# A fused attention and two-layer feed-forward kernel: GpSimd alone makes the fold's forms, and the big output stage's small operations are reordered

## The reference

```
x = attention(q, mean of k over 8, mean of v over 8)      # 2304 tokens x 512
x = x / rms(x) * rms_g
h = silu(x @ w_gate) * (x @ w_val)                        # 512 -> 1536, FFN 1
x = h @ w_out                                             # 1536 -> 512
out = silu(x @ w2_in) @ w2_out                            # 512 -> 2048 -> 512, FFN 2
```

## Time and profile before

| | us |
|---|---|
| median of 3 runs | 895.41 (895.05 to 895.97) |
| profiled execution, its own time | 899.02 |
| its span, first to last instruction | 897.2 |
| TensorE busy | 872.5 |
| VectorE busy | 520.8 |
| ScalarE busy | 356.9 |
| GpSimd busy | 336.5 |

### The profile page before, as it was taken

The page is one execution under the profiler, slowest core; times in us unless marked ns, Lnnn a source line. Parts: engine busy times, 40 slices in busy tenths (PEclk is TensorE's granted clock), DMA queues, the critical chain, the costliest instruction groups (busy, mean ns, idle before and its releaser), DMA issues.

```text
span 897.2 us, 12951 instructions
## 1 busy us (share of the span) xinstructions
PE 872.5 (97%) x4896; PEld 828.2 (92%) x4896; DVE 520.8 (58%) x831; ACT 356.9 (40%) x671; POOL 336.5 (38%) x345
## 2 busy tenths in 40 slices
PE   7999999999989999999999999998999999999998
PEld 6899999999889999999898999898989998989897
DVE  6689757765456766655654355668555544433433
ACT  3679744542243432355453212134234332322222
POOL 6898999883254422568771000314000000000000
PEclk9999999999999999999999999999999999999999
DMA  9971777766999984756779286765764545474321
GB/s 267 259 199 35 276 268 287 282 274 216 409 349 399 395 291 160 256 207 233 300 298 359 83 313 247 266 224 196 299 224 165 191 172 201 176 281 176 129 93 71
DMA packets 64716, 213.69 MB, mean 238 GB/s; under 512 B 22288, under 2 KB 32528, under 8 KB 51472
## 3 DMA queue, kind: packets, MB, share of 16 engines
q1 hardware_dynamic: 64656, 212.88, 65.5%
HBM read 145.75 MB, written 67.11 MB: 237 GB/s over the span
## 4 chain that ended last, share of the span: by engine, by line
PE 87%; DMA 5%; POOL 3%; DVE 2%; SPq 1%; issue 1%; ACT 1%; DVEq 0%; ACTq 0%; POOLq 0%
PE ps L1672 15%; PE ps L1674 15%; PE ps L1673 15%; PE ps L1741 7%; PE ps L1742 7%; PE ps L1740 7%; PE ps L1601 3%; PE ps L1716 3%; PE ps L1715 3%; PE ps L1714 3%; DMA raw_c<-in_moe_w_out 2%; PE ps L1769 2%; PE ps L1770 2%; PE ps L1771 2%; PE ps L1572 2%; DMA raw_x<-in_moe_w_out 1%
## 5 line engine op out<-in xcount | busy, mean ns | idle before, releaser
L1672 PE MATMUL ps<-xh,wr 128*128 128x384 f32 x840 | 284.4, 339 | 9.6 <-DVE vt L1320 6.7
L1674 PE MATMUL ps<-xh,wr 128*128 128x384 f32 x840 | 282.9, 337 | 0.0
L1673 PE MATMUL ps<-xl,wr 128*128 128x384 f32 x840 | 282.4, 336 | 0.0
L1672 PEld LDWEIGHTS ps<-xh,wr 128*128 128x128 f32 x840 | 158.7, 189 | 14.0 <-DVE vt L1320 7.7
L1673 PEld LDWEIGHTS ps<-xl,wr 128*128 128x128 f32 x840 | 158.8, 189 | 0.9
L1674 PEld LDWEIGHTS ps<-xh,wr 128*128 128x128 f32 x840 | 158.6, 189 | 0.0
L1742 PE MATMUL ps<-wo,al 128*128 128x512 f32 x288 | 112.5, 391 | 0.0
L1741 PE MATMUL ps<-wo,ah 128*128 128x512 f32 x288 | 112.4, 390 | 0.0
L1740 PE MATMUL ps<-wo,ah 128*128 128x512 f32 x288 | 112.0, 389 | 0.0
L1015 ACT ACTIVATE ah<-qt 128x384 fp32r<-128x384 f32 x96 | 45.0, 517 | 131.2 <-PE ps L1742 126.5
L1357 DVE TENSOR_TENSOR al<-qt,ah 128x384 fp32r<-128x384 f32 x96 | 51.9, 582 | 72.6 <-ACT ah L1015 72.4
(11 more groups left out here) (172 smaller groups left out, 1388.1 us busy)
## 6 DMA issues: line engine op xcount, KB each, us to landing
wr<-ring_home SPq DMA_DIRECT2D x40, 1792.0 KB, 8.6
ring_home<-wr SPq DMA_DIRECT2D x20, 1792.0 KB, 8.1
wo<-out_home SPq DMA_DIRECT2D x22, 1024.0 KB, 4.9
out_home<-wo SPq DMA_DIRECT2D x14, 1024.0 KB, 9.7
fw<-fold_home SPq DMA_DIRECT2D x7, 1536.0 KB, 6.3
raw_c<-in_moe_w_out SPq DMA_DIRECT2D x19, 512.0 KB, 8.2
fold_home<-fb SPq DMA_DIRECT2D x6, 1024.0 KB, 10.2
fold_home<-fa SPq DMA_DIRECT2D x6, 768.0 KB, 6.9
```

Source lines behind the costliest of these rows:

```text
L1672: pe.matmul(out_ps, w_hi, x_hi, start=first and c == 0, stop=False, skip_group_check=True)
L1673: pe.matmul(out_ps, w_hi, x_lo, start=False, stop=False, skip_group_check=True)
L1674: ins = pe.matmul(out_ps, w_lo, x_hi, start=False, stop=c == 1, skip_group_check=True)
```

## The change

It has two parts.

- The fold. ScalarE makes none of it. GpSimd copies the high parts itself (`fold_raw`, and the copy inside `fold_sums`). `a` and `b` of one piece follow each other and share one raw load (`raw_x`, `raw_y`), so six loads of 512 KB go. All twelve entries come in phase 1, two pieces a group, in its groups 0 to 2: SP keeps an even piece at the group's value unit, an odd one at the next gate unit (`a`) and the down after it (`b`). `wo` of down 5 is made in the place where b0 was. `token_high` of phase 2's forms 2 to 4 moves one group later, since `raw_x` and `raw_y` lie on their space, and waits for b4 and b5.
- The big stage and what is around it. `form_high(0)` is a unit earlier on ScalarE; the three parts of `form_low(0)` come one each in units 39, 40 and 41 where all three came in unit 40. The first product waits for gating 1 of unit 43 where it waited for gating 3; the third waits for gating 2. The sums for form 6 go from GpSimd to VectorE. Low parts come ahead of token sums, and the token work moves up to one product later. In units 44 and 45 the high and low parts of down 26 come between the silus and sums, one block of them already in unit 44.

The diff, less blank lines, distant context and the declaration of a semaphore `s_fold`:

```diff
@@ -139,7 +139,9 @@
-        return [C22, C12, C11, C21] if ffn_of[n - 1] == 1 and classic[n - 1] else [C11, C21, C22, C12]
+        if classic[n - 1]:
+            return [C22, C12, C11, C21] if ffn_of[n - 1] == 1 else [C11, C21, C22, C12]
+        return SILUS
@@ -153,7 +155,7 @@
-    HIGH_AT = {1: {2: (0, 1), 3: (2, 3, 4), 4: (5, 6)}, 2: {2: (0, 1), 3: (2, 3), 4: (4, 5), 5: (6,)}}
+    HIGH_AT = {1: {2: (0, 1), 3: (2, 3, 4), 4: (5, 6)}, "late": {2: (0, 1), 3: (2,), 4: (3, 4, 5, 6)}, 2: {2: (0, 1), 3: (2, 3), 4: (4, 5), 5: (6,)}}
@@ -162,8 +164,8 @@
-    WLOW_AT = [[], [0, 1, 2], [3, 4], [5], [6, 7], [8, 9], [10]]
-    WHIGH_AT = [[], [0], [1, 2], [3], [4, 5], [6], []]
+    WLOW_AT = [[], [0, 1], [2, 3], [4], [5, 6], [7, 8], [9, 10]]
+    WHIGH_AT = [[], [], [0], [1, 2], [3, 4], [5], [6]]
@@ -177,16 +179,19 @@
-        if g == GROUPS[1] - 1:
-            made.append(("b", 0))
         made.append(("o", g))
+    for j in range(2 * PART):
+        made += [("a", j), ("b", j)]
     FOLD_AT = {}
-    for g in range(5):
-        entries = [("a", 2 * g), ("b", g + 1), ("a", 2 * g + 1)] if g < 3 else [("b", g + 1)]
-        made += entries
-        for what, entry in zip(("gate", "down", "value") if g < 3 else ("down",), entries):
-            FOLD_AT[what, g] = entry
+    for j in range(2 * PART):
+        g = j // 2
+        places = [("unit", 2 * GROUPS[1] + 2 * g + 1)] * 2
+        if j % 2:
+            places = [("unit", 2 * GROUPS[1] + 2 * g + 2), ("down", GROUPS[1] + g)]
+        for entry, place in zip((("a", j), ("b", j)), places):
+            FOLD_AT.setdefault(place, []).append(entry)
@@ -214,9 +219,9 @@
-        if kind in "ob":
+        if kind == "o":
             return 2
-        if kind == "a":
+        if kind in "ab":
@@ -226,9 +231,9 @@
-    raw_count = [sum(1 for j in range(i + 1) if raw_of(j) == raw_of(i)) for i in range(len(made))]
+    raw_count = [sum(1 for j in range(i + 1) if raw_of(j) == raw_of(i) and made[j][0] != "b") for i in range(len(made))]
     sums0 = [3 * sum(1 for m in made[:i] if m[0] in "rb") for i in range(len(made) + 1)]
-    his0 = [sum({"r": 3, "a": 2}.get(m[0], 1) for m in made[:i]) for i in range(len(made) + 1)]
+    his0 = [sum({"r": 3, "o": 1}.get(m[0], 0) for m in made[:i]) for i in range(len(made) + 1)]
@@ -487,7 +493,7 @@
-                if raw_next[i] is not None and made[raw_next[i]] != ("r", U2 + 1):
+                if raw_next[i] is not None and made[raw_next[i]] != ("r", U2 + 1) and made[raw_next[i]][0] != "b":
@@ -574,19 +580,13 @@
-                if item == ("unit", 10):
-                    keep(made_at["b", 0])
-                if item == ("unit", 12):
+                if item == ("unit", first_unit[1]):
                     load_raw(made_at["a", 0])
                     load_raw(made_at["a", 1])
-                if kind == "down" and ("gate", x - last_down[0]) in FOLD_AT:
-                    keep(made_at[FOLD_AT["gate", x - last_down[0]]])
-                if kind == "unit" and units[x][0:2] == (1, "V"):
-                    for what in ("down", "value"):
-                        if (what, units[x][2]) in FOLD_AT:
-                            keep(made_at[FOLD_AT[what, units[x][2]]])
-                    if units[x][2] == 4:
-                        load_raw(made_at["r", U2 + 1])
+                for entry in FOLD_AT.get(item, []):
+                    keep(made_at[entry])
+                if item == ("unit", last_unit[1] - 2):
+                    load_raw(made_at["r", U2 + 1])
@@ -604,8 +604,8 @@
-                if item in (("unit", 9), ("unit", 11)):
-                    keep(made_at["o", 4 + (x == 11)])
+                if item in (("unit", 9), ("unit", 10)):
+                    keep(made_at["o", x - 5])
@@ -731,33 +731,42 @@
+            def fold_raw(i):
+                j = made[i][1]
+                r = raw[raw_of(i)][:, :].rearrange("p (k n) -> p k n", k=2)
+                if j:
+                    pool.wait_ge(s_ast, 16 * j)
+                else:
+                    pool.wait_ge(s_prod, NF * (last_unit[0] + 1))
+                pool.wait_ge(s_raw[raw_of(i)], 16 * raw_count[i])
+                pool.tensor_copy(fa[:, 0:2, 0, :], r[:, :, 0:FF])
+                pool.tensor_copy(fa[:, 2, 0, :], r[:, 1, FF:2 * FF]).then_inc(s_fold, 1)
+                pool.wait_ge(s_fold, 2 * j + 1)
+                pool.tensor_tensor(fa[:, 0:2, 1, :], r[:, :, 0:FF], fa[:, 0:2, 0, :], ALU.subtract)
+                pool.tensor_tensor(fa[:, 2, 1, :], r[:, 1, FF:2 * FF], fa[:, 2, 0, :], ALU.subtract).then_inc(s_wlo, 1)
...
+                j = made[i][1]
                 r = raw[raw_of(i)][:, :].rearrange("p (k n) -> p k n", k=2)
...
                 s1, s2, s3, s4 = [fbt[:, f, 1, :] for f in range(4)]
-                if made[i] == ("b", 0):
+                if j:
+                    pool.wait_ge(s_bst, 16 * j)
+                else:
                     pool.wait_ge(s_wlo, made_at["r", last_unit[0]] + 1)
-                else:
-                    pool.wait_ge(s_bst, 16 * made[i][1])
-                pool.wait_ge(s_raw[raw_of(i)], 16 * raw_count[i])
                 pool.tensor_tensor(s1, a21, a22, ALU.add).then_inc(s_ws, 1)
...
-            def fold_low(i):
-                r = raw[raw_of(i)][:, :].rearrange("p (k n) -> p k n", k=2)
-                pool.wait_ge(s_whi, his0[i + 1])
-                if made[i][0] == "a":
-                    pool.tensor_tensor(fa[:, 0:2, 1, :], r[:, :, 0:FF], fa[:, 0:2, 0, :], ALU.subtract)
-                    pool.tensor_tensor(fa[:, 2, 1, :], r[:, 1, FF:2 * FF], fa[:, 2, 0, :], ALU.subtract)\
-                        .then_inc(s_wlo, 1)
-                else:
-                    pool.tensor_tensor(fb[:, 0:2, 1, :], fbt[:, 0:2, 1, :], fb[:, 0:2, 0, :], ALU.subtract)
-                    pool.tensor_tensor(fb[:, 2:4, 1, :], fbt[:, 2:4, 1, :], fb[:, 2:4, 0, :], ALU.subtract)\
-                        .then_inc(s_wlo, 1)
+                pool.wait_ge(s_ws, sums0[i] + 3)
+                pool.tensor_copy(fb[:, :, 0, :], fbt[:, :, 1, :]).then_inc(s_fold, 1)
+                pool.wait_ge(s_fold, 2 * j + 2)
+                pool.tensor_tensor(fb[:, 0:2, 1, :], fbt[:, 0:2, 1, :], fb[:, 0:2, 0, :], ALU.subtract)
+                pool.tensor_tensor(fb[:, 2:4, 1, :], fbt[:, 2:4, 1, :], fb[:, 2:4, 0, :], ALU.subtract).then_inc(s_wlo, 1)
@@ -767,13 +776,10 @@
-                elif f == 5:
+                else:
                     pool.wait_ge(s_ft, j + 1)
...
                     pool.tensor_tensor(b12, b22, b12, ALU.subtract).then_inc(s_ft, 1)
-                else:
-                    pool.wait_ge(s_flo, 2 * PART + j + 1)
-                    pool.tensor_tensor(b11, b21, b11, ALU.subtract).then_inc(s_ft, 1)
@@ -844,25 +850,16 @@
-                else:
-                    if made[i] == ("b", 0):
-                        fold_sums(i)
-                    fold_low(i)
-                    if made[i][0] == "a" and made[i][1] % 2:
-                        fold_sums(made_at["b", made[i][1] // 2 + 2])
-                    elif made[i] == ("b", 4):
-                        fold_sums(made_at["b", 5])
-                if made[i] == ("o", last_down[0]):
-                    fold_sums(made_at["b", 1])
+                elif made[i][0] == "a":
+                    fold_raw(i)
+                else:
+                    fold_sums(i)
...
                 hidden_sums(5, j)
-            for j in range(PART):
-                hidden_sums(6, j)
@@ -896,19 +893,6 @@
-                    return
-                if kind == "a":
-                    r = raw[raw_of(i)][:, :].rearrange("p (k n) -> p k n", k=2)
-                    if x:
-                        act.wait_ge(s_ast, 16 * x)
-                    else:
-                        act.wait_ge(s_prod, NF * (last_unit[0] + 1))
-                    act.activation(fa[:, 0:2, 0, :], r[:, :, 0:FF], ACT.Copy).then_inc(s_whi, 1)
-                    act.activation(fa[:, 2, 0, :], r[:, 1, FF:2 * FF], ACT.Copy).then_inc(s_whi, 1)
-                    return
-                if kind == "b":
-                    act.wait_ge(s_ws, sums0[i + 1])
-                    act.activation(fb[:, :, 0, :], fbt[:, :, 1, :], ACT.Copy).then_inc(s_whi, 1)
@@ -948,11 +932,13 @@
-                        act.wait_ge(s_wlo, made_at["a", 2 * PART - 1] + 1)
+                        act.wait_ge(s_wlo, made_at["b", 2 * PART - 2] + 1)
                     src = forms(p, *((0, 0), (1, 0), (1, 1))[f])
...
                     src = xt[XHOME[b]][:, f - 3, :, :]
+                    if b == 2 and f == 3:
+                        act.wait_ge(s_wlo, made_at["b", 2 * PART - 1] + 1)
@@ -1040,10 +1026,10 @@
-                    if f in (3, 5, 6):
-                        act.wait_ge(s_ft, (3, 5, 6).index(f) * PART + j + 1)
-                    elif f == 4:
-                        act.wait_ge(s_ft2, j + 1)
+                    if f in (3, 5):
+                        act.wait_ge(s_ft, (3, 5).index(f) * PART + j + 1)
+                    elif f in (4, 6):
```

(58 more changed lines are left out.)

## The result

The changed kernel takes 887.09 us (median of 4 runs, 886.6 to 888.5) against 895.69 us (4 runs): ratio 0.9902, 95% interval 0.9882 to 0.9923. It is 8.6 us faster where 11.9 were forecast, inside the range. The profiled execution took 888.49 us with a span of 886.5.

A forecast was written before the change was run, and what follows sets the result against it. TensorE bounds the kernel (busy 872.5 of 897.2 us); only its waits and slow-clock time can be won. Terms 1.2 + 3.9 + 1.45 + 4.5 + 1.1 - 0.3 = 11.9 us took 895.4 to 883.5 us, range 875.5 to 889.0.

The forecast's parts named there:

- The three gaps around unit 11 to 13 go: Units 11 to 13: freeing ScalarE from the fold removes three TensorE gaps and one slow stretch, 7.9 us.
- The chain of `b` entries, its pitch and b5: Fold on GpSimd: 7.0 us work plus store landing, pitch 14.6 us, b5 made at 320.2.
- Rival 2: Fold: GpSimd's copies cost the two-input price, pitch 16.3 us, b5 at 331; 894.5 us, chance 0.07.
- A new stall at down 9 and cover at down 8: Down 8's output weights land in time; down 9 waits 5.0 us plus 1.7 slow, leaving 1.2 us net gain.
- Traffic says the same: Fold groups: 9.4 MB needs 24.0 us at 393 GB/s, while TensorE passes a group in 22.9 us.
- Low parts one to a unit: Units 40 to 42: unit 41's 2.22 us gap and its slow stretch go, 3.9 us, less 0.3 for a late sum.
- start of the big stage: First product waits for gating 1 of unit 43, not gating 3: 1.45 us go.
- its fourth product: Big stage: form 6's sums on VectorE and low parts first remove a 2.77 us gap and slow stretch, 4.5 us.
- unit 45: Units 44 and 45: low parts interleaved with silus start sooner, so a 1.08 us gap goes, counted 1.1.
- The order of low parts and token sums: Big stage: low parts come ahead of token sums, counted with the moved sums in one 4.5 us gain.
- From the profile to the median: Whole kernel: the 11.9 us saving from the 899.0 us profiled execution carried to the 895.4 median, giving 883.5.
- Rival 1: Down 9: no new stall, loads landing faster, b5 by 315; 18.6 us saved, 876.8 us, chance 0.28.

The follow-up runs named there:

- fold_only: Kernel before with only the fold half of the change, big stage and units 39 to 45 as before: 897.23 us, ratio 1.0001 to before.
- repaced: Changed kernel with stores b2 to b5 and a3 to a5 moved to later items of SP's queue: 880.15 us, ratio 0.9808 to before.
- stage_only: Kernel before with only the change's big stage and units 39 to 45, fold as before: 887.58 us, ratio 0.9893 to before.
- start_gating3: Changed kernel with the big stage's first product waiting for gating 3 again: 890.14 us, ratio 0.9923 to before.
- sums6_on_pool: Changed kernel with the three subtractions for form 6 back on GpSimd, order as changed: 893.51 us, ratio 0.9953 to before.
- tokens_first: Changed kernel with token sums ahead of low parts in the big stage, form 6's sums left on VectorE: 887.73 us, ratio 0.9907 to before.
- the repeat: The changed kernel itself, unaltered, measured once more beside the kernel before: 888.15 us, ratio 0.9889 to before.
- wo_first: Changed kernel with the next output weights' load ahead of the b store in SP's queue at downs 6 to 8: 892.33 us, ratio 0.9946 to before.
- wo_ring_first: Changed kernel with output-weight loads and, in units 13, 15, 17, ring loads ahead of b stores in SP's queue: 887.36 us, ratio 0.9885 to before.
- first_and_late: Changed kernel with output-weight and ring loads ahead of b stores and phase 2's token forms one group later: 888.36 us, ratio 0.9895 to before.
- late_only: Changed kernel with phase 2's token forms one group later, SP's queue as in the change: 891.95 us, ratio 0.9933 to before.

## Why the prediction was right, and what was off

- *The three gaps around unit 11 to 13 go, 7.9 us.* Right: unit 14 begins 8.7 us earlier in the profile (246.5 against 255.2); the step left out gaps too small for the earlier trace rows.
- *The chain of `b` entries, its pitch and b5.* Right as a mean, 14.7 against 14.6 us, b5 kept at 319.2 against 320.2. That it fits so closely is in part luck: the work on an entry takes 7.4 us (b4, from 299.1 to 306.5) where 7.0 were reckoned, the landing and hand-over 7.3 on average where 7.6 were, and the single steps are up to 2 us off. The estimate from the Trainium skill (GPSIMD Engine Reference, section Elementwise — side-by-side cycle accounting) was 0.88 us for the 1024 copy; the trace has 1.04 us at least and 1.08 as a mean. The shortest copies take 0.40, 0.61 and 1.04 us for 256, 512 and 1024 elements, which makes 0.83 ns an element and some 0.19 us fixed, an estimate from these three; the fixed part is what both estimates lacked. Rival 2, the two-input price, is out. The rule that the prediction put on its side, from the Trainium skill (GPSIMD Engine Reference, section Engine selection), did not speak for it: its row gives the factor of two for two-input operations and calls one-input ones roughly line-rate, and the trace agrees, 1.04 against 2.5 us.
- *A new stall at down 9 and cover at down 8.* Half right, and this is the step that failed: "`wo` for down 8 leaves after b3 (291.0), lands 8.4 us later at 299.4, and is needed at 308.6 - 7.9 = 300.7". It left at 293.0 and landed 10.1 us later, at 303.1, and TensorE was there at 299.9. The step had counted only the `b` store ahead of the load. Left out were the raw load in front of that store, 0.52 MB, the 1.3 us that SP needed to issue the store, and the rest of a ring load that was under way until 295.3. At down 9, where no raw load stands in front, it was a ring load again, under way until 324.6, and `wo` took 9.9 us in place of 8.4. No run separates these shares. In place of one stall of 5.0 us with 1.7 behind it, 6.7, came two, 3.3 and 1.75 us, each with its stretch, 8.5. Net of the fold part: 1.2 us forecast, 0.0 measured (`fold_only`, 1.0001).
- *Traffic says the same.* This second reason for the stall does not hold. `repaced` moves the same bytes with no late load, and in the changed kernel the DMA engines stood nearly idle (share 0.03) right behind the first stall, while SP still stood at b4. The stall came from SP's order, which the first reason had right.
- *Low parts one to a unit, 3.9 us less 0.3; start of the big stage, 1.45; its fourth product, 4.5; unit 45, 1.1.* Right together: 10.65 us forecast; the span gained 10.7 in the profile with nothing left from the fold, and `stage_only` measured 9.6 (0.9893). Only `start_gating3` and `sums6_on_pool` test a term by itself; for units 41 and 45 the profile shows that the gap is gone. The 0.3 us came, since from unit 24 to the big stage 5.0 us were saved and not 5.4, but the trace points to another cause than the one given: in units 40 and 42 TensorE has small delays, and there a gating on VectorE took 1.92 us in place of 0.55, while GpSimd's subtraction ran beside it. No run tests it.

```profile
563.97 1.92 DVE L1329 TENSOR_TENSOR hid<-qt,vt 128x384 f32<-128x384 f32 x1
```

```profile
563.62 1.85 POOL L778 TENSOR_TENSOR hid<-hid 128x768 f32<-128x768 f32 x1 [79.58 <-DVE fl L1356]
```

- *The order of low parts and token sums.* It was counted together with the moved sums; `tokens_first` shows that the sums alone did it.
- *From the profile to the median.* The saving of one profiled pair was carried over whole. Between the profiled executions it was 10.5 us, between the medians 8.6. The profiled execution of before stood 3.3 us over its median of 895.69 and that of after 1.4; this accounts for 1.9 of the 3.3 us by which the forecast was too high, the failed step for 1.2 more. The 1.9 us are no more than the uncertainty: the interval of the 8.6 us is 6.9 to 10.6, and the repeat gave 10.0 (0.9889).
- *Rival 1*, no new stall, 876.8 us. For the change as it was made it is out: the stalls came, and b5 was not there by 315. `repaced` reaches its time in another way, by the order of the queue with b5 at 319.3: 1.9% under before, where the rival had 2.1%.

## What to carry to other kernels

Work that leaves a critical engine is paid for where its results are handed on: the queue that stores them waits in order, and a load behind such a wait is late even where the engines have room for it. Place each store in the transfer queue at the time at which its producer, at its real pitch (its work plus the landing of the store that frees its buffer), has it made; moving loads ahead of stores only shifted the wait to the next entry here (`wo_first`, `wo_ring_first`, `first_and_late`). And where GpSimd and VectorE both run operations with two SBUF inputs at once, count their slowing of each other before their busy time.

## What the runs showed of the hardware that was not expected

- It looks as if GpSimd and VectorE do not share in small steps; no run here tests that by itself. A VectorE operation with two SBUF inputs beside a GpSimd one of the same kind took about as long as that one (1.92 for 0.55 us beside 1.85; three low parts 7.47 for 2.7 us beside 10.1), and GpSimd's three took 10.1 and 9.3 us where three at 1.85 make 5.5. The Trainium skill (GPSIMD Engine Reference, section Key points) names the contention, and that section gives no price; the trace agrees, and these rows have one.
- Every stretch at the lower clock level in the profiles came behind a gap, but the length of the gap alone tells neither whether one comes nor how long it is. A gap of 1.75 us ahead of down 9 had one of 3.4 us in the changed kernel, 1.67 us ahead of down 8 in its repeat had none. The 2.2 us in unit 41 had one in the kernel before and none in `fold_only`. A gap of 3.45 us had 6.8 us at half clock in the repeat, as gaps of 3.3 to 3.6 us had in `wo_ring_first`, `sums6_on_pool` and `late_only`, where 3.46 and 3.47 us in `tokens_first` and `first_and_late` had 3.4. And in `late_only` a gap of 3.52 us ahead of down 8 had none. The repeat's window behind its longer gap:

```profile
329.20:335.20 6.00, 6.00 (x19) 6.00 (x20) 0.02 (x1) 0.45 (x1) 0.00 (x0) 0.50 1.01 431
```

and `late_only` behind its gaps of 3.52 and 3.28 us:

```profile
303.00:306.00 3.00, 2.73 (x15) 2.73 (x16) 0.00 (x0) 0.00 (x0) 2.86 (x4) 1.00 0.05 19
329.70:336.40 6.70, 6.66 (x23) 6.66 (x24) 0.52 (x1) 0.00 (x0) 0.00 (x0) 0.55 1.02 436
```

So the 1.7 us for a slow stretch that a sum adds to each gap is a chance and not a constant.
